# Moving the spreads of the value means from SyncE's queue to ScalarE's, and three extra TensorE matmuls at the start of the kernel

## The reference

```python
def _attn_ref(q, k, v):                      # 2 x 8 heads, 768 tokens, 64 features, float32
    block, window = (32, 16)
    k_sum = k.reshape(B, H, nb, block, D).max(axis=3)
    v_sum = v.reshape(B, H, nb, block, D).mean(axis=3)
    scores_l = scale * (q @ k.T), kept where |i - j| < window, else -1e9
    scores_s = scale * (q @ k_sum.T) + log(block)
    a = softmax(concatenate([scores_l, scores_s]))
    return a @ concatenate([v, v_sum])

def _moe_ref(x, w_in, w_out):                # 1536 tokens, 512 -> 2048 -> 512
    h = maximum(x @ w_in, 0); return (h * h) @ w_out

def _moe2_ref(x, w_in, w_out, a, b):
    h = x @ w_in
    P = a[0] + a[1] * h + a[2] * h**2 + a[3] * h**3
    Q = 1 + |b[0]| * |h| + |b[1]| * h**2
    return (P / (Q + 1e-6)) @ w_out
```

## Time and profile before

| | |
|---|---|
| median of 3 runs | 622.24 us (619.99 to 626.68) |
| profiled execution | 619.3 us, span 617.2 us, mean granted clock 0.999 |
| PE | 581.2 us busy (94%) |
| DVE | 443.0 us (72%) |
| ACT | 261.6 us (42%) |
| POOL | 147.2 us (24%) |
| start of the last output of the attention (L519) | 85.44 us |

### The profile page before, as it was taken

One profiled execution on the slowest core, in us unless ns is written; L12 is line 12 of the kernel. 1 busy time (PEld: TensorE's weight loads), 2 busy tenths in 40 slices (PEclk: granted clock), 3 DMA queues, 4 the chain that ended last, 5 costly groups with the idle time before them and its releaser, 6 DMA issues.

```text
span 617.2 us, 9768 instructions
## 1 busy us (share of the span) xinstructions
PE 581.2 (94%) x3360; PEld 473.0 (77%) x3360; DVE 443.0 (72%) x839; ACT 261.6 (42%) x556; POOL 147.2 (24%) x158
## 2 busy tenths in 40 slices
PE   4587899999999999999999989999999999999995
PEld 3465678888888888888888867788888888888884
DVE  5467798765343333356765699999999999999996
ACT  4477731110131110311110855566766566766564
POOL 6255640000030000120000566622222222222220
PEclk9999999999999999999999999999999999999999
DMA  8477544000000000023322200000100000100001
GB/s 252 100 212 246 191 163 184 0 1 0 1 1 0 0 0 0 0 68 103 103 102 102 69 1 0 1 0 1 68 0 0 0 0 0 69 1 0 1 1 68
DMA packets 13535, 32.55 MB, mean 53 GB/s; under 512 B 1728, under 2 KB 4416, under 8 KB 13504
## 3 DMA queue, kind: packets, MB, share of 16 engines
q1 hardware_dynamic: 13360, 31.99, 16.1%
q10 hardware_dynamic: 144, 0.13, 0.1%
HBM read 27.79 MB, written 3.15 MB: 50 GB/s over the span
## 4 chain that ended last, share of the span: by engine, by line
PE 46%; DVE 35%; issue 9%; ACT 3%; DMA 3%; SPq 2%; DVEq 1%; POOL 0%; POOLq 0%
PE bank L533 22%; PE bank L585 21%; DVE ratio L981 9%; DVE numer L963 6%; DVE ratio L975 5%; DVE numer L961 5%; DVE ratio L970 5%; DVE hhi L988 4%; DMA kraw<-kT 3%; ACT prob L665 2%; SPq L262 1%; PE bank L502 1%; PE bank L519 1%; DVE hlo L992 1%; PE bank L483 1%
## 5 line engine op out<-in xcount | busy, mean ns | idle before, releaser
L533 PE MATMUL bank<-xhi,whi 128*128 (+1 forms) x384 | 149.8, 390 | 0.1
L533 PE MATMUL bank<-xhi,wlo 128*128 (+1 forms) x384 | 149.4, 389 | 0.0
L533 PE MATMUL bank<-xlo,whi 128*128 (+1 forms) x384 | 149.4, 389 | 0.0
L443 POOL TENSOR_TENSOR denom<-denom,habs 128x512 f32<-128x512 f32 (+1 forms) x49 | 62.3, 1273 | 251.0 <-ACT denom L736 251.0
L678 ACT ACTIVATE hsq<-bank 128x512 f32<-128x512 f32 x48 | 28.8, 600 | 213.2 <-PE bank L533 213.1
L533 PEld LDWEIGHTS bank<-xhi,whi 128*128 128x128 f32 x384 | 72.1, 188 | 15.2 <-issue 0.3
L533 PEld LDWEIGHTS bank<-xhi,wlo 128*128 128x128 f32 x384 | 72.1, 188 | 15.1
L533 PEld LDWEIGHTS bank<-xlo,whi 128*128 128x128 f32 x384 | 72.1, 188 | 14.7
L600 PE MATMUL bank<-whi,hhi 128*128 128x512 f32 x192 | 75.9, 395 | 7.6 <-DVE hlo L992 7.6
L600 PE MATMUL bank<-wlo,hhi 128*128 128x512 f32 x192 | 74.8, 390 | 0.0
L600 PE MATMUL bank<-whi,hlo 128*128 128x512 f32 x192 | 74.8, 390 | 0.0
(11 more groups left out here) (69 smaller groups left out, 862.2 us busy)
## 6 DMA issues: line engine op xcount, KB each, us to landing
wraw<-w SPq DMA_DIRECT2D x32, 512.0 KB, 4.1
vwin<-vw SPq DMA_DIRECT2D x16, 288.0 KB, 5.4
q<-qT SPq DMA_DIRECT2D x8, 384.0 KB, 6.0
out<-osb SPq DMA_DIRECT2D x12, 256.0 KB, 2.1
kraw<-kT SPq DMA_DIRECT2D x7, 384.0 KB, 6.1
vwin<-vsum SPq DMA_DIRECT2D x32, 36.0 KB
kraw<-kT SPq DMA_DIRECT2D x2, 128.0 KB, 2.4
kraw<-kT ACTq DMA_DIRECT2D x1, 128.0 KB, 2.7
```

The lines of the kernel that those rows point to most:

```text
L443: g.tensor_tensor(denom[:, i, cols], denom[:, i, cols], habs[:, i, cols], ALU.mult).then_inc(q_done, 1)
L533: last = mm(hps[j % 2][:, :], W[a][:, j, kt * P:(kt + 1) * P], X[b][:, kt, bass.ds(CH * c, CH)], start=kt == 0 and i == 0, stop=kt == KT - ...
```

## The change

Three things change in the source.

1. The function `spread_summary` leaves SyncE's program and goes to ScalarE's, where it issues one transfer, (n, t), at a time. `exps` gets a list of such pairs and issues one after each of its activations. The spread of block 0 goes out in exps(2); those of blocks 1 and 2 in one `exps` each, four transfers in a row of four activations; those of blocks 3 to 7 in two successive `exps`, two transfers each. If there are four, the signal `exp_done` goes out ahead of the fourth transfer.
2. SyncE's program is written as a plain loop: queries of block n, keys of block n + 1, values of block n, and the first weights; the coefficients and the weights of slots 3 to 7 come after the loop. The keys of block 1 now come ahead of the values of block 0. The summary of block 2 moves from group 3 to group 4.
3. VectorE clears the tile probT[0] as its first instruction, and TensorE then multiplies that tile with itself WARM = 3 times (128 columns against 512), into the bank of the summaries, ahead of its first scores. Nothing reads the result.

```diff
--- before.py
+++ after.py
@@ -65,8 +65,9 @@
 XPAIRS = GROUPS // 2
 KP = S + 2 * BAND
 THIRD = S // GPB
+WARM = 3
 SPLIT_FROM = GROUPS - 7
-SUMMARY_AT = [0, 1, 3] + [GPB * n - 4 for n in range(3, NB)]
+SUMMARY_AT = [0, 1, 4] + [GPB * n - 4 for n in range(3, NB)]
 
 
 def unit(j, h):
@@ -180,6 +181,7 @@
     mask_step = sem("mask_step")
     means_clear, means_done = sem("means_clear"), sem("means_done")
     edges = sem("edges")
+    idle_clear = sem("idle_clear")
     coef_step = sem("coef_step")
 
     ksum_done = sem("ksum_done")
@@ -254,15 +256,6 @@
             for half in (slice(0, NW // 2), slice(NW // 2, NW)):
                 sp.dma_start(vwin[n % V_RING][0:KW, half, :], vw[n][:, half, :]).then_inc(vw_in[n % V_RING], 16)
 
-        def spread_summary(n):
-
-            sp.wait_ge(vsum_copied, n + 1)
-            for t in range(4):
-                rows = KW + 2 * GPB * t
-                sp.dma_start(vwin[n % V_RING][rows:rows + 2 * GPB, :, :],
-                             vsum[n % 2][32 * t:32 * t + 2 * GPB, :].unsqueeze(1).to_broadcast([2 * GPB, NW, P])
-                             ).then_inc(vsum_in[n % V_RING], 16)
-
         def load_first(j):
             sp.dma_start(wraw[:, j:j + 1, :], w1[j:j + 1].rearrange("a p n -> p a n")).then_inc(w_first, 16)
 
@@ -274,37 +267,19 @@
         load_k_first(0)
         load_k_first(2)
         load_q(0)
+        load_k(1)
         load_vwin(0)
-        load_k(1)
-        load_q(1)
-        load_k(2)
-        load_vwin(1)
-        load_q(2)
-        for n in range(NB):
-            if n == 0:
-                load_vwin(2)
-            elif n + RING < NB:
-                load_vwin(n + RING)
-            if n + RING < NB:
-                load_k(n + RING)
-            if n == 0:
-                spread_summary(0)
-                load_vwin(RING)
-                spread_summary(1)
-            if n + RING < NB:
-                load_q(n + RING)
-            if 2 <= n < 2 + EARLY:
-                load_first(n - 2)
-            if n == 5:
-                sp.dma_start(ca[:, :], coef_a.partition_broadcast(P)).then_inc(coef_in, 16)
-                sp.dma_start(braw[:, :], coef_b.partition_broadcast(P)).then_inc(coef_in, 16)
-            if n >= 5:
-                for j in range(EARLY + 2 * (n - 5), min(EARLY + 2 * (n - 4), FT // 2)):
-                    load_weights(w1, j, *landing(j))
-            if n == 1:
-                spread_summary(2)
-            if 0 < n and n + 2 < NB:
-                spread_summary(n + 2)
+        for n in range(1, NB):
+            load_q(n)
+            if n + 1 < NB:
+                load_k(n + 1)
+            load_vwin(n)
+            if RING <= n < RING + EARLY:
+                load_first(n - RING)
+        sp.dma_start(ca[:, :], coef_a.partition_broadcast(P)).then_inc(coef_in, 16)
+        sp.dma_start(braw[:, :], coef_b.partition_broadcast(P)).then_inc(coef_in, 16)
+        for j in range(EARLY, FT // 2):
+            load_weights(w1, j, *landing(j))
         sp.wait_ge(o_done, done(2, GROUPS - 1))
         with sp.Fori(0, FT // 2 // LAND) as k:
             for i in range(LAND):
@@ -553,6 +528,9 @@
 
         early = {GROUPS - 4: [(0, 0), (0, 1)], GROUPS - 3: [(0, 2), (1, 0)],
                  GROUPS - 2: [(0, 3), (1, 1)], GROUPS - 1: [(1, 2), (1, 3)]}
+        pe.wait_ge(idle_clear, 1)
+        for _ in range(WARM):
+            mm(vps[:, :], probT[0][:, 0:P], probT[0][:, :], start=True, stop=True)
         pe.wait_ge(consts, 4)
         scores(0)
         scores(1)
@@ -658,13 +636,28 @@
             last = a.copy(means[:, j, 2 * j:2 * j + 2], mean[:, :])
         last.then_inc(means_done, 1)
 
-        def exps(G, r):
+        def exps(G, r, spreads=()):
 
             act.wait_ge(s_free, done(2, G))
             for u in range(GU):
                 last = a.activation(prob[r][:, u, :], prob[r][:, u, :], ACT.Exp, bias=lowest[r][:, u:u + 1],
                                     scale=-1.0, accum_out=rowsum[r][:, u:u + 1])
-            last.then_inc(exp_done, 1)
+                if u < len(spreads):
+                    if u == GU - 1:
+                        last.then_inc(exp_done, 1)
+                    spread_summary(*spreads[u])
+            if len(spreads) < GU:
+                last.then_inc(exp_done, 1)
+
+        def spread_summary(n, t):
+
+            act.wait_ge(vsum_copied, n + 1)
+            if n >= V_RING:
+                act.wait_ge(o_done, done(2, GPB * (n - V_RING + 1) - 1))
+            rows = KW + 2 * GPB * t
+            act.dma_start(vwin[n % V_RING][rows:rows + 2 * GPB, :, :],
+                          vsum[n % 2][32 * t:32 * t + 2 * GPB, :].unsqueeze(1).to_broadcast([2 * GPB, NW, P])
+                          ).then_inc(vsum_in[n % V_RING], 16)
 
         def copy_summary(n):
             act.wait_ge(vsum_done, n + 1)
@@ -680,13 +673,22 @@
         exps(0, 0)
         exps(1, 1)
         copy_summary(0)
-        exps(2, 2)
+        exps(2, 2, [(0, t) for t in range(4)])
         for G in range(GROUPS):
+            spreads = []
+            for n in range(1, NB):
+                first = SUMMARY_AT[n] + 1
+                if n < RING and G == first:
+                    spreads = [(n, t) for t in range(4)]
+                elif n >= RING and G == first:
+                    spreads = [(n, 0), (n, 1)]
+                elif n >= RING and G == first + 1:
+                    spreads = [(n, 2), (n, 3)]
             act.wait_ge(t_done, done(P_RING, G))
             act.wait_ge(o_done, done(2, G - 2))
             a.copy(probT[G % 2][:, :], tps[0:COLS, :]).then_inc(probT_done, 1)
             if G + 3 < GROUPS:
-                exps(G + 3, (G + 3) % P_RING)
+                exps(G + 3, (G + 3) % P_RING, spreads)
             if G == GROUPS - 2:
                 relu(0, 0)
             for n in range(1, NB):
@@ -785,6 +787,7 @@
         dve.sem_inc(xlo_done, 2)
         dve.sem_inc(g_ready, 2)
 
+        d.memset(probT[0][:, :], 0.0).then_inc(idle_clear, 1)
         for r in range(RING):
             d.memset(kraw[r][:, 0:BAND], 0.0)
             last = d.memset(kraw[r][:, BAND + S:], 0.0)
```

## The result

| | before | changed |
|---|---|---|
| median | 622.68 us (619.99 to 626.68, 4 runs) | 641.28 us (640.29 to 644.02, 4 runs) |
| profiled execution | 619.3 us, span 617.2 us | 642.22 us, span 640.5 us |
| mean granted clock | 0.999 | 0.965 |

The change makes the kernel slower: ratio 1.030, 95% interval 1.023 to 1.037. The forecast of 615.5 us and its range, 608 to 624, were wrong, and so was the sign. The medians differ by 18.6 us and the two profiled executions by 22.9: the profiled one of before was 3.4 us faster than its median, so what follows, read from the profiles, shows a little more than the typical loss.

The account below looks back on a forecast made before the run. In mid-stage attention no engine is full; key loads issued late behind spreads hold up the blocks. 619.3 - 4.5 + 2.5 - 3.4 = 613.9, put halfway to the median: 615.5 us, range 608 to 624.

Parts of the forecast that it names:

- The first spread: Block 0's spread, on ScalarE's own queue, lets output(0) start at 17.5 us (bounds 17 and 22): gain 4.5 us.
- blocks 1 and 2: Spreads issued one group later: output(3) still 10.3 us after output(0), output(6) about 10.1 after output(3) instead of 7.58, loss 2.5.
- block 7 and the weights: From 71.03 us: earlier weight loads compete with spreads, but late landings have about 1.4 us to spare; counted as 0.
- ScalarE's issues: Blocks 3 to 6: of two issues the first hides, the second costs 0.4 to 0.5 us; 0.25 per issue, block of 7.5.
- Rival D: ScalarE stands still 0.77 us per issue between the activations of exps: slower, 625.6 us; chance 0.15.
- SyncE's term: Blocks 3 to 6: SyncE, free of spreads, issues keys earlier; VectorE's 8.4 us of waits go, gain 3.4 us.
- The matmuls: Three early TensorE matmuls end at 5.0 us, hidden before the first scores; nothing taken for the scores, at most 2.4 us lost.
- Rival C: The queue doesn't matter: the first spread lands at 22 us as before, the rest as forecast, 618.4 us; chance 0.18.

Follow-up runs that it names:

- wide packets: The changed kernel with the summary written four times side by side, so spread packets have 2,048 B instead of 512: 634.98 us, ratio 1.022.

## Why the prediction was wrong

**The step that failed is "The first spread".** It took 17.5 for output(0), "since 36 KB transfers can then pass loads of 384 KB that only queue in the other ring". They do not pass. The spread's first packet left 1 us sooner than before, and then its packets went one for one with the loads': output(0) at 27.4 instead of 17.5, which is beyond both ends of the bound (17 and 22). The own queue gave no head start either: the first packet left at 17.1 here, and at 17.3 from SyncE's queue in the kernel with the keys early. The end of 22 took the one queue of before as the worst case; but one queue, where the spread's packets came behind the loads and then took turns with none (3.2 us), is the better case here. The nearest row that I had the earlier trace rows had only two loads beside it; I noted that and still leaned on it.

**The same step was used three times more, without saying so.** "Landing 2.3 after that", plus 0.8 for loads, stands in blocks 1 and 2; outputs 3 and 6 came 14.5 and 14.4 us after their predecessors instead of 10.3 and 10.1. "A late landing has about 1.4 us to spare" stood in for block 7 and the weights; 14.8 us from output(12) to output(15) show what that was worth. The text itself named landings of over 5 us on ScalarE's queue as what would break the forecast. Against the 613.9 of the sum, the first spread is 9.9 us off, block 1 4.2, block 2 4.3, and the block before output(15) 7.3 (14.8 less 7.5): 25.7 of the 28.3 us to 642.2. Not all of it is landing. Output(0) to output(1) took 4.5 us and output(3) to output(4) 4.4, where the sum had 2.7: 1.8 and 1.7 us of the excess of blocks 1 and 2 are work at 1.2 GHz behind the wait before. And 0.8 us of the first term are issues that began later than forecast.

**ScalarE's issues were right.** 0 for the first of a pair and 0.42 for the second, 0.21 per issue against 0.25. Only where four stand in one group did ScalarE lose more, 2.2 us in exps(2). Rival D, ScalarE standing still, did not happen; the right sign of D would have come for a wrong reason.

**SyncE's term was right where a spread was in time.** No wait of VectorE for keys is left, and the three groups from 66.56 take 7.35 us against 7.5. Over output(6) to output(12) that saved 0.8 us, before one late spread took it back. The change moved two things, and the useful one did not need the other: keys one turn earlier on SyncE's own queue gain 6.9 us, more than the 3.4 that the sum had for this term.

**The matmuls** were forecast at next to nothing and are: 622.08 against 622.05 us alone. They ended at 6.3, not 5.0, and the first scores began at 6.54 instead of 5.92 but took 1.05 instead of 1.88 us.

**Rival C** had the mechanism nearest to right, and was too kind: it let the first spread land as before. By the Trainium skill ("DMA: Bandwidth & Descriptors", section "Issuing engines are not separate DMA queues"), all issuers' transfers interleave on the same engines. The trace agrees, 27 spread packets beside some 70 load packets each us; I gave it 4.5 us and a chance of 0.18. Interleaved like this, a transfer can come out later than it would from the back of one queue: 26.6 here, 21.2 before. That case, with SyncE's earlier loads as what it interleaves with, was the missing rival on the slow side.

**What stays open.** Why the first packet of block 0 leaves 5.4 us after the issue was not isolated. A busy share near 1 is not the whole of it: 1.4 us were enough at a share of 0.77 (block 2) and at 0.87 (last spread of before), against 1.04 in block 0. That delay and the pauses between transfers stayed with wide packets, which brought 6.3 us and not more. Of the clock I can only say that it fell during three of the four long waits and that 1.2 GHz followed all four, which made each late spread dearer than its wait.

## What to carry to other kernels

Before a small transfer that others wait for is given a queue of its own, ask what else the DMA engines carry at that time: behind the loads of one queue it waits once, beside the loads of another it may pay for a load's packet at each of its own. A bound for a landing under load must come from a landing under load, and its upper end must allow for more than before. And if an in-order issuer holds up an urgent load behind a waiting transfer, first try to move that load ahead of the wait, which took a few lines here and gave 1.2% (0.4 to 2.0%).

## What the runs showed of the hardware

- Two queues on the same DMA engines shared them about one packet for one, and not in long groups: a bunch of six to eight spread packets of 512 B every 0.23 us beside load packets of 3,072 B and every 0.11 us beside load packets of 1,536 B, and of six of 2,048 B every 0.3 us beside 3,072 B. That a bunch is one packet for each of six engines is read from its size and from the six completion records; the records name no engine.
- The first spread, issued at a DMA share of 1.04 with many loads issued ahead of it, sent its first packet after 5.4 us; later ones sent theirs after 1.4 us, at shares of 0.28 to 0.87.
- An issue on ScalarE (0.75 us, the very first 1.38) overlaps activations already handed over; of two in a group only the second showed, mostly as 0.42 us; of the first four the gaps were 1.06, 0.38, 0.36 and 0.41 us.
- TensorE's granted clock fell to 0.5 in stretches in kernels with long waits, but also from 50.3 to 57.2 us in the kernel with nothing but the three matmuls added, where the median stayed the same. Around that fall TensorE waited 1.36 and 1.39 us, where in the kernel before it waited 0.54 and 1.39. The 1.00 that the earlier trace rows give for the clock ahead of 26 us is no reading: the first clock record in the trace of before is at 26.05, and the durations say 1.2 GHz up to there.
